# 96 instead of 94 rows of local keys and values, the mask's second part earlier, and all first loads on one queue in order of need

## The reference

```
scores_l = where(|i - j| < 16, scale * q @ k.T, -1e9)            # local
scores_s = scale * q @ k_sum.T + log(32)                          # 24 summaries
a        = softmax(concat[scores_l, scores_s]); x = a @ concat[v, v_sum]
```

## Time and profile before

| | |
|---|---|
| median of 3 runs | 526.18 us (525.91 to 526.33) |
| the profiled execution | 526.93 us, span 525.1 us |
| TensorE busy (matmul) | 488.1 us, 93% of the span |
| VectorE, ScalarE, GpSimd busy | 249.2, 210.3, 49.9 us |
| mean granted TensorE clock | 0.971 of full speed |
| DMA traffic | 37.27 MB, mean 71 GB/s |

### The profile page before, as it was taken

One profiled execution on the slowest core, in us unless ns is written; L12 is line 12 of the kernel. 1 busy time (PEld: TensorE's weight loads), 2 busy tenths in 40 slices (PEclk: granted clock), 3 DMA queues, 4 the chain that ended last, 5 costly groups with the idle time before them and its releaser, 6 DMA issues.

```text
span 525.1 us, 8265 instructions
## 1 busy us (share of the span) xinstructions
PE 488.1 (93%) x3144; PEld 440.2 (84%) x3144; DVE 249.2 (47%) x497; ACT 210.3 (40%) x549; POOL 49.9 (9%) x75
## 2 busy tenths in 40 slices
PE   7178199999899999999999999999999999999997
PEld 6166089898799999999999999999988888888885
DVE  4236355576964444445444324445656344444430
ACT  2246345655454333434343323333444223433331
POOL 2013123241320000000000000000000000000000
PEclk9669779999999999999999999999999999999999
DMA  8514941233214001004100022122122100000011
GB/s 298 181 65 126 327 173 32 88 89 91 69 38 131 21 20 30 28 18 146 30 23 1 1 76 87 40 81 68 53 75 67 61 21 21 20 21 20 21 39 41
DMA packets 26262, 37.27 MB, mean 71 GB/s; under 512 B 2116, under 2 KB 16180, under 8 KB 26224
## 3 DMA queue, kind: packets, MB, share of 16 engines
q1 hardware_dynamic: 25408, 34.50, 20.5%
q10 hardware_dynamic: 816, 2.25, 1.2%
HBM read 30.30 MB, written 6.29 MB: 70 GB/s over the span
## 4 chain that ended last, share of the span: by engine, by line
PE 80%; SPq 9%; DVE 4%; DMA 2%; ACT 2%; issue 2%; DVEq 0%; ACTq 0%
PE bank L844 25%; PE bank L871 23%; PE bank L990 11%; PE bank L963 11%; SPq L265 4%; SPq L247 4%; PE bank L786 3%; PE bank L801 2%; DMA mask<-mask_c 2%; PE bank L833 2%; PE bank L978 2%; ACT probs L423 1%; SPq L250 1%; DVE solu L743 0%; DVE stat L735 0%
## 5 line engine op out<-in xcount | busy, mean ns | idle before, releaser
L844 PE MATMUL bank<-x_hi,win_hi 128*128 128x384 f32 x256 | 89.4, 349 | 0.0
L844 PE MATMUL bank<-x_lo,win_hi 128*128 128x384 f32 x256 | 86.5, 338 | 0.0
L844 PE MATMUL bank<-x_hi,win_lo 128*128 128x384 f32 x256 | 86.5, 338 | 0.0
L871 PE MATMUL bank<-h_hi,wout_hi 128*128 128x384 f32 x256 | 85.7, 335 | 0.0
L871 PE MATMUL bank<-h_hi,wout_lo 128*128 128x384 f32 x256 | 85.6, 334 | 0.0
L871 PE MATMUL bank<-h_lo,wout_hi 128*128 128x384 f32 x256 | 85.6, 334 | 0.0
L638 DVE TENSOR_TENSOR sqr<-relu 128x384 f32<-128x384 f32 x64 | 37.5, 586 | 99.8 <-ACT relu L477 99.5
L477 ACT ACTIVATE relu<-bank 128x384 f32<-128x384 f32 x64 | 31.5, 492 | 113.4 <-PE bank L844 113.4
L844 PEld LDWEIGHTS bank<-x_hi,win_hi 128*128 128x128 f32 x256 | 48.5, 190 | 4.0 <-issue 3.4
L844 PEld LDWEIGHTS bank<-x_lo,win_hi 128*128 128x128 f32 x256 | 48.7, 190 | 0.0
L844 PEld LDWEIGHTS bank<-x_hi,win_lo 128*128 128x128 f32 x256 | 48.6, 190 | 0.0
(11 more groups left out here) (79 smaller groups left out, 740.2 us busy)
## 6 DMA issues: line engine op xcount, KB each, us to landing
win_raw<-w_in_t SPq DMA_DIRECT2D x8, 512.0 KB, 12.6
wout_raw<-w_out_t SPq DMA_DIRECT2D x8, 512.0 KB, 12.6
win_raw<-w_t SPq DMA_DIRECT2D x8, 512.0 KB, 3.6
v_ext<-vwin SPq DMA_DIRECT2D x24, 141.0 KB
out<-o_sb SPq DMA_DIRECT2D x12, 256.0 KB, 2.0
k_raw<-kT SPq DMA_DIRECT2D x7, 399.0 KB, 5.8
q_sb<-qT SPq DMA_DIRECT2D x24, 96.0 KB, 2.1
v_next<-vblk SPq DMA_DIRECT2D x4, 384.0 KB, 6.4
```

Source lines behind the costliest of these rows:

```text
L844: last = nc.tensor.matmul(up_bank(n), win[a][:, f * WC + k * P:f * WC + (k + 1) * P], x[b][:, c % 2, k * CH:(k + 1) * CH], start=(k == 0 a ...
L871: last = nc.tensor.matmul(down_bank(d), wout[a][:, f * WC + d * P:f * WC + (d + 1) * P], h[b][:, n % 3, :], start=(f == 0 and a == 0 and b ...
```

## The change

The window becomes 96 rows wide: the last two columns of a tile are masked keys (the mask marks them as out of reach). `KX` becomes 120, and the padded keys and values get 800 positions where they had 798. ScalarE issues no DMA any more; SP issues all in one order, and the mask's second part goes between `v_ext_first`'s second part and the first `w_out` request. TensorE's wait for `ident` moves from `turned(0)` to `means(0)`.

```diff
-WIN = QT + 2 * MARGIN
+WIN = QT + 2 * MARGIN + 2
+SE = S - QT + WIN
-        k_raw = sb(att, "k_raw", [P, PPB, S + 2 * MARGIN], F32)
+        k_raw = sb(att, "k_raw", [P, PPB, SE], F32)
...
+            def load_q_first(h):
+                sp.dma_start(q_first[:, h, :], q_head[h, :, :]).then_inc(qf_in[h], 16)
+
             load_k(0, 0)
+            load_q_first(0)
             sp.dma_start(mask[:, 0:UC + KX], mask_c[:, 0:UC + KX]).then_inc(mask_in, 16)
+            load_k(0, 1)
             load_k(0, 2)
+            load_vf(0)
+            sp.dma_start(ident[:, :], ident_c).then_inc(ident_in, 16)
             load_k(0, 3)
+            load_vw_first(0)
             load_vf(1)
-            sp.dma_start(q_first[:, 1, :], q_head[1, :, :]).then_inc(qf_in[1], 16)
+            load_vf(2)
+            load_q_first(1)
             load_w(win_raw, w_in_t, 0, win_in)
             load_vf(3)
             load_vw_first(1)
+            sp.dma_start(mask[:, UC + KX:], mask_c[:, UC + KX:]).then_inc(edge_in, 16)
             load_w(wout_raw, w_out_t, 0, wout_in)
...
             load_w(win_raw, w_in_t, 2, win_in)
-            sp.dma_start(mask[:, UC + KX:], mask_c[:, UC + KX:]).then_inc(edge_in, 16)
             sp.dma_start(g_sb[:, :], g_cols).then_inc(g_in, 16)
...
-            act.dma_start(q_first[:, 0, :], q_head[0, :, :]).then_inc(qf_in[0], 16)
-            act.dma_start(k_raw[:, 1, :], kT[1, :, :]).then_inc(k_in[1], 16)
-            act.dma_start(ident[:, :], ident_c).then_inc(ident_in, 16)
-            act.dma_start(v_first[:, 0, :], vrows[0, :, :]).then_inc(vf_in[0], 16)
-            act.dma_start(v_ext_first[NB:KX, 0, :], vwin_head[0, :, :]).then_inc(vwf_in[0], 16)
-            act.dma_start(v_first[:, 2, :], vrows[2, :, :]).then_inc(vf_in[2], 16)
```

More of the change, by code:

```diff
@@ L792, in turned @@
             def turned(u):
-                if u == 0:
-                    pe.wait_ge(ident_in, 16)
                 pe.wait_ge(norm_ok, u + 1)
@@ L804, in means @@
             def means(p):
+                if p == 0:
+                    pe.wait_ge(ident_in, 16)
                 pe.wait_ge(vf_in[p], 16)
@@ L1011 @@
     q_units = by_unit(pairs_T(q).reshape(B * PPB, P, RB, UQ).swapaxes(1, 2))
-    k_pad = np.zeros((B * PPB, P, S + 2 * MARGIN), np.float32)
+    k_pad = np.zeros((B * PPB, P, SE), np.float32)
     k_pad[:, :, MARGIN:MARGIN + S] = pairs_T(k)
     v_pairs = v.reshape(B * PPB, 2, S, D).transpose(0, 2, 1, 3).reshape(B * PPB, S, P)
-    vp = np.zeros((B * PPB, S + 2 * MARGIN, P), np.float32)
+    vp = np.zeros((B * PPB, SE, P), np.float32)
     vp[:, MARGIN:MARGIN + S] = v_pairs
```

## The result

The changed kernel takes 503.72 us (median of 4 runs, 502.98 to 505.14) against 526.24 us: ratio 0.9576, 95% interval 0.9554 to 0.9599. The profiled execution took 503.33 us, with a span of 501.5. The forecast was 502.0, range 498.3 to 505.5.

The account below looks back on a forecast made before the run. TensorE's own work bounds the main loop; only the stretch ahead, with two DMA waits, can give much. 16.15 + 8.06 + 0 + 0.4 - 0.4 = 24.2 us off 526.93 gives 502.7, or 502.0 against the median; range 498.3 to 505.5.

Parts of the forecast that it names:

- The values' windows: At values(0) to turned(2): with 96 rows the 13.8 us DMA wait goes, turned(2) starts 16.15 us earlier.
- From there to scores(8): From turned(2) to scores(8): engines repeat what they did, so scores(8) goes from 51.06 to 34.9 us.
- The mask's rest: At maxima(8): its whole 8.06 us wait for the mask's second part goes; the 6.44 us chain to scores(9) stays.
- The clock at the loop's start: First loop step from scores(9): TensorE's clock falls again in the lull before it, so 2.74 us are not gained.
- the forecast's case: Before scores(9): the clock falls in the 4.8 us lull, so 0 of 2.74 us is gained.
- my two cases: At the loop's start: clock falls, 502.0 us (chance 0.50), or clock stays up, 499.2 us (chance 0.32).
- One queue: At the start: first keys land sooner with all requests on SP, 0.4 us gained, ends -0.3 and +0.9.
- Wider tiles: In every unit's scores and the first chains: two more columns cost 0.4 us, ends 0.2 and 0.8.
- my own case: Whole kernel: the forecast of 502.0 us, its own range 501 to 503.5, chance 0.50.
- a late transfer: First 40 us: slower DMA rates make values(0) wait 3 us; 505 us, band 503.5 to 508, chance 0.09.
- Does not spread: Values' windows: 96 rows stay on two DMA engines, scores(9) at about 50; 510 us, chance 0.07.
- the slower case: Before scores(8): one slow queue delays all, at 100 GB/s scores(9) some 15 us later; 541 us, chance 0.01.

Follow-up runs that it names:

- e1_rows94: The changed kernel with 94 rows again, keeping one queue, its order and the mask's early place: 517.21 us.
- e4_rows95: The changed kernel with windows of 95 rows instead of 96: 509.07 us.
- e5_width_alone: The kernel before with 96 rows and nothing else changed (two queues, mask's second part late in the list): 502.91 us.
- e3_two_queues: The changed kernel with the first requests on two queues in the old order, six of them from ScalarE, mask early: 504.29 us.
- e7_window_first: The changed kernel with windows_k(9) ahead of w_in_low(3) on GpSimd: 499.10 us.
- e2_mask_late: The changed kernel with the mask's second part back in its late place, ahead of g_sb: 504.63 us.
- e10_short_warmup: The changed kernel with 4 instead of 6 products on zeros ahead of scores(0): 503.69 us.
- e12_scores8_early: e9_window_first_filled with scores(8) directly behind values(7), six products sooner, and fill(5) for fill(11): 496.67 us.
- e8_filled: The changed kernel with products of no use in TensorE's idle times, around values(4) and values(5), after the last up(1) and before scores(9): 500.35 us.
- e9_window_first_filled: The changed kernel with windows_k(9) ahead of w_in_low(3) and useless products around values(4), values(5) and before turned(8): 497.82 us.

## Why the prediction was right, step by step

**The values' windows: right in mechanism and size.** 16.15 us forecast at `turned(2)`, 16.37 measured. It includes the clock: two `means` took 2.80 us warm (granted clock 1.0), 5.01 cold (0.5). The cause, the engine count, was an inference from one share; `e1_rows94`, `e4_rows95` and `e5_width_alone` show it. The transfers were slower than I reckoned, which the margins hid: part 0 landed at 13.6 us where I had 11.3 to 12.3, the mask's rest at 23.2 where I had 19.8 to 20.8. And I had put the 305 GB/s of 10 to 15 us down to the two busy engines; with 96 rows the same stretch has 304.

**From there to scores(8): one term missed.** I wrote that the engines repeat what they did. They did, but the clock did not. It fell at about 30 us, after a stretch in which TensorE was busy 3.08 of 5 us, and `scores(8)` stood at 15.11 instead of 16.37 us gained: 1.26 us lost. I had looked for lulls only behind `scores(8)`. Whether the clock falls there differs between executions: in `e5_width_alone`, `e3_two_queues` and `e7_window_first` TensorE was busy 2.94, 3.08 and 3.10 us of the same 5 and the clock stayed up, while it fell in `e2_mask_late` (2.94) and `e10_short_warmup` (3.04). So the busy time of the stretch does not tell it, and what does stays open. With the clock up `scores(8)` came at 34.86 in `e5_width_alone`, my 34.9.

**The mask's rest: right in the profile, wrong as a part of its own.** 8.06 forecast, 7.61 measured (15.42 us from `scores(8)` to `scores(9)` became 7.81). The 0.45 is `maxima(8)`: I let it start 0.1 us after the scores, and it starts 0.51 after them in this kernel and in `e12_scores8_early`. That the early place was needed to remove the wait, as my text treats it, is refuted: late in the list with 96 rows it is in time too. I had both halves of this before me, SP's 16.78 us in one issue and the five weight requests ahead of the mask, and did not ask when SP would reach it once the held issue was gone.

**The clock at the loop's start: the forecast's case, at half its price.** It fell in the lull, at about 43.6, and had risen by 47.1. The first step took 6.68 us from `scores(9)`; before it was 7.86, and warm 5.12. So 1.18 of the 2.74 were gained. Which part of the loss a run gets varies (the first step took 6.69 us in `e5_width_alone`, 7.33 in `e2_mask_late`, 7.93 in `e3_two_queues`), and my two cases, 502.0 and 499.2, should have been one with a spread.

**One queue: 0.4 forecast, 0.15 in this execution, nothing in the medians.** The first keys landed 1.24 us earlier, more than the 0.9 of my bound, but the 12 products on zeros, which had ended at 5.40 before, ended at 6.40, and `scores(0)` started at 6.33 instead of 6.48. I had not listed TensorE's own work as the next thing late. How long these products take differs between executions. Where they took 4.33 to 4.98 us with one queue (`e2_mask_late`, `e8_filled`, `e9_window_first_filled`, `e12_scores8_early`), `values(0)` came at 15.12 to 15.23 us; with two queues (`e3_two_queues`, `e5_width_alone`) at 15.70 and 15.71. So the order gives up to 0.6 us at that place, and the medians, 504.29 with two queues and 503.72 with one, are too wide to tell it.

**Wider tiles: 0.4 forecast, 0.3 measured** from the end of the first step to the end: 450.8 us in all three profiled executions with 94 rows, 451.1 to 451.2 in all with 96.

The sum: 16.37 (with the queue's part in it) - 1.26 + 7.61 + 1.18 - 0.30 = 23.60, against 24.2 forecast. That it comes so close is in part luck: a fall of the clock that I did not see (-1.26) and half a fall less than I had put in (+1.18) nearly cancel. The median lies 0.4 above the profiled execution where it was 0.7 below it before, which is the rest of the 1.7 us between 502.0 and 503.72. The 503.72 lies just above the band that I gave my own case (501 to 503.5), and in the band of a late transfer (503.5 to 508), though no transfer was late.

**The rivals.** "Does not spread" was mispriced: 510, with `scores(9)` at about 50; made so in `e1_rows94` it was 517.21, with `values(0)` 4 us later than reckoned, the clock down behind both waits, and `scores(9)` at 57.54. No other DMA wait of TensorE came, and the slower case had nothing for it.

## What to carry to other kernels

Read the DMA share where requests are open and engines wait: a floor of 0.12 is two engines of sixteen, and two more rows of masked padding (0.3 us) freed 23. Such engines also hold up the requests behind and the issuing queue, so a second late transfer (here the mask) can be the same fault; ask when the queue would reach it once the first is gone. When a long stall goes, look through the whole compressed stretch for new lulls in TensorE's work, not only at the next wait, and price the clock as a spread.

## What the runs showed that I had not expected

- In `e7_window_first` the clock fell at about 41.1 us, over a microsecond after TensorE had gone back to work at 39.89, behind an idle time of 2.15 us. If the one brought the other, which no run here separates, an idle time can be paid for in the work behind it.

```profile
40.00:41.00 1.00, 1.00 (x15) 1.00 0.98 223
41.00:42.00 1.00, 1.00 (x7) 0.57 1.05 236
```

- The same 12 products on zeros at the start took 4.30 to 5.49 us in the twelve profiled executions that have them, with the clock listed as 1.00 (4.30 us in the kernel before, 5.31 in the changed one). Work at the start can be slow without the clock column saying so.
- Some 0.5 us lie between the end of `scores(8)` and `maxima(8)`, where `scores(0)` to `maxima(0)` has 0.1. What it is stays open.
